# Expert stage: the relu rows change partition quarters through memory, and the second product runs two tiles behind the first

## The reference

```
logits = x @ w_gate;  expert = argmax(logits);  gate = softmax(logits)[expert]
for e in range(8):
    xe  = x[tokens of e]                      # rows gathered by expert
    h   = maximum(xe @ w1[e], 0)              # 512 -> 1024
    out[tokens of e] = gate * (h @ w2[e])     # 1024 -> 512
```

## Time and profile before

| what | value |
|---|---|
| median of 3 runs | 1513.52 us (1509.26 to 1514.18) |
| the profiled execution, its own time | 1509.39 us |
| its span, first to last instruction | 1507.7 us |
| PE busy | 98% of the span |
| DVE, ACT, POOL busy | 65%, 47%, 42% |
| expert stage, first product of tile 3 to the end | 1058.6 to 1507.7 us |

### The profile page before, as it was taken

The page is one execution under the profiler, slowest core; times in us unless marked ns, Lnnn a source line. Parts: engine busy times, 40 slices in busy tenths (PEclk is TensorE's granted clock), DMA queues, the critical chain, the costliest instruction groups (busy, mean ns, idle before and its releaser), DMA issues.

```text
span 1507.7 us, 28846 instructions
## 1 busy us (share of the span) xinstructions
PE 1473.6 (98%) x8070; PEld 1274.8 (85%) x8071; DVE 979.4 (65%) x1877; ACT 713.0 (47%) x1512; POOL 630.7 (42%) x681
## 2 busy tenths in 40 slices
PE   7999999999999999999999999999999899999997
PEld 6999999999978888888888888887888778888885
DVE  5688888888825374655637465535677777777663
ACT  5688788788812122121212212143566566656442
POOL 6676676676810021020202102021667776665221
PEclk9999999999999999999999999999999999999999
DMA  7354344344430202021120202134424433321110
GB/s 254 115 142 107 104 107 107 103 108 127 109 122 0 71 15 84 0 84 28 56 70 14 84 0 84 29 131 153 167 96 141 163 116 130 125 73 49 40 48 23
DMA packets 84601, 134.67 MB, mean 89 GB/s; under 512 B 50016, under 2 KB 50272, under 8 KB 80338
## 3 DMA queue, kind: packets, MB, share of 16 engines
q1 hardware_dynamic: 76978, 114.01, 25.2%
q0 software_dynamic: 7584, 20.17, 4.2%
HBM read 104.26 MB, written 30.94 MB: 90 GB/s over the span
## 4 chain that ended last, share of the span: by engine, by line
PE 67%; DVE 1%; DMA 1%; POOL 1%; issue 1%; ACT 1%; POOLq 0%; ACTq 0%; DVEq 0%
PE bank L166 65%; PE bank L1669 1%; POOL big L1104 1%; DVE xs L1466 1%; DMA arena<-rows_scratch,ids 1%; ACT arena L1244 0%; DMA out<-arena,ids 0%; DVE arena L1451 0%; PE bank L1600 0%; PE bank L1705 0%; PE bank L1619 0%; PE bank L1608 0%; ACT big L809 0%; PE bank L1594 0%; DVE xs L1428 0%
## 5 line engine op out<-in xcount | busy, mean ns | idle before, releaser
L166 PE MATMUL bank<-big,xs 128*128 (+1 forms) x2088 | 492.6, 395 | 14.7 <-DVE big L609 8.1
L166 PEld LDWEIGHTS bank<-big,xs 128*128 128x128 f32 x2088 | 391.7, 189 | 96.7 <-issue 15.8
L166 PE MATMUL bank<-xs,big 128*128 128x512 f32 x1728 | 397.4, 391 | 2.7 <-PEq L215 2.7
L166 PEld LDWEIGHTS bank<-xs,big 128*128 128x128 f32 x1728 | 324.7, 188 | 70.3 <-issue 2.9
L166 PE MATMUL bank<-big 128*128 128x512 f32 (+1 forms) x1632 | 325.8, 348 | 2.0 <-POOL big L305 1.4
L166 PEld LDWEIGHTS bank<-big 128*128 128x128 f32 (+1 forms) x1632 | 255.8, 165 | 36.2 <-POOL big L305 1.7
L1021 POOL TENSOR_TENSOR arena<-arena 128x512 f32<-128x512 f32 x32 | 39.8, 1255 | 440.5 <-DMA arena<-rec_scratch 440.2
L1397 DVE TENSOR_TENSOR arena<-arena,bank 128x512 f32<-128x512 f32 x72 | 49.4, 686 | 246.0 <-PE bank L166 246.0
L1157 ACT COPY arena<-bank 128x512 f32<-128x512 f32 x72 | 42.3, 587 | 306.9 <-PE bank L166 302.6
L1322 DVE CUSTOM_DVE_ANT_0 arena<-arena 128x512 f32<-128x512 f32 x256 | 159.5, 688 | 14.9 <-ACT arena L1177 14.7
L1451 DVE TENSOR_SCALAR arena<-bank,gate 32x256 f32<-32x256 f32 x288 | 138.9, 482 | 44.5 <-PE bank L166 40.1
(11 more groups left out here) (175 smaller groups left out, 1395.0 us busy)
## 6 DMA issues: line engine op xcount, KB each, us to landing
arena<-we SPq DMA_DIRECT2D x32, 1024.0 KB, 4.8
kqraw<-kq SPq DMA_DIRECT2D x32, 576.0 KB, 3.8
rows_scratch<-arena SPq DMA_DIRECT2D x36, 256.5 KB
xT_scratch<-arena SPq DMA_DIRECT2D x32, 288.0 KB
arena<-v SPq DMA_DIRECT2D x64, 128.0 KB, 2.4
arena<-xT_scratch SPq DMA_DIRECT2D x8, 1024.0 KB, 5.4
arena<-rec_scratch SPq DMA_DIRECT2D x64, 128.0 KB, 3.8
arena<-w3T SPq DMA_DIRECT2D x8, 512.0 KB, 3.4
```

Of the source, the lines that this page charges most:

```text
L166: ins = nc.tensor.matmul(out, left[a], right[b], start=first and n == 0, stop=last and n == 2)
```

## The change

The relu is again one instruction per half on ACT, with partitions in place. `relu_stored(g)` then stores the 128 x 1024 rows to a scratch tensor in HBM (512 KB, one DMA issued by ACT), and `load_quarters(g)`, later in ACT's tile, waits for the store and issues four loads of 128 KB, each of 32 partitions x (4 x 256 columns), which bring the quarters to their places in `hq`. DVE turns the rows of tile g - 1 in tile g, and PE's second product in tile g is that of g - 2. The weight subtraction of the loop moves from POOL to DVE, at the end of DVE's tile; POOL's tile is a gather and a scatter. ACT's chunks move to the end of its tile, behind the loads. The table of chunks is worked out anew for the longer distance. In the prologue second product(1) and the transposes of tile 2 go; in the tail PE makes first product(39), second product(37) with the transposes of tile 39 between its halves, `last_product` (tile 39, its parts in buffers of its own), and then second product(38).

```diff
+            def relu_stored(g):
+                for h in range(2):
+                    relu_half(g, h, True)
+                act.wait_ge(relu_done[0], g + 1)
+                act.dma_start(m["hrows"][ds(g * P, P), :], hs).then_inc(h_stored, 16)
+
+            def load_quarters(g):
+                act.wait_ge(h_stored, 16 * g + 16)
+                stored = m["hrows"][ds(g * P, P), :].rearrange("(b i) (a c) -> a i b c", i=Q, a=P // Q)
+                for a in range(P // Q):
+                    act.dma_start(hq[a * Q:(a + 1) * Q, :].rearrange("i (b c) -> i b c", b=P // Q), stored[a]
+                                  ).then_inc(hq_in, 16)
...
             def tile(g):                       # ACT
-                relu_moved(g)
+                relu_stored(g)
                 rows_high(g + 1, False)
+                next_gate(g + 1)
+                turned_h_high(g - 1)
+                load_quarters(g)
                 tile_chunks(act, g, weights)
-                next_gate(g + 1)
-                turned_h_high(g)
...
             def tile(g):                       # DVE
-                relu_moved(g)
-                turn_h(g)
-                result(g - 1)
-                turned_h_low(g)
+                rows_low(g + 1)
+                turn_h(g - 1)
+                result(g - 2)
+                turned_h_low(g - 1)
+                tile_chunks(dve, g, weights)
...
             def period(g):                     # POOL
                 gather(g + 2)
-                tile_chunks(pool, g, weights)
-                scatter(g - 1)
+                scatter(g - 2)
...
             def tile(g):                       # PE
-                here, before = weights_of(g), weights_of(g - 1)
+                here, before = weights_of(g), weights_of(g - 2)
                 for h in range(2):
                     first_product(g, h, *here)
                 x_transpose(g + 1)
-                second_product(g - 1, *before)
+                second_product(g - 2, *before)
...
+            pe.wait_ge(ht_lo, 2)               # PE, prologue
             h_transpose(1)
 
             for h in range(2):
                 first_product(2, h, 0, 0)
             x_transpose(3)
-            second_product(1, 0, 0)
-            h_transpose(2)
+            second_product(0, 0, 0)
...
-            second_product(g1, *before, between=lambda: h_transpose(g))
-            second_product(g, *here, out=ylast_ps, left=htlast)
+            second_product(g2, *before2, between=lambda: h_transpose(g))
+            last_product(*here)
+            second_product(g1, *before)
```

More of the change, by code:

```diff
@@ L110, in alloc @@
     over("filler", [XW], xs_at)
[L111 removed]
+    over("htlast", [2, FF // 2], arena_at + (SLOTS * CW + FF) * 4, F32R)
     def cut(*parts):
@@ L1111, in _ @@
             pool.wait_ge(tabs, 2)
[L1112 to L1115, removed]
             def period(g):
                 gather(g + 2)
-                tile_chunks(pool, g, weights)
-                scatter(g - 1)
+                scatter(g - 2)
             last = tiles(pool, period, 2)
-            last1, last2 = last_of(pool, 1), last_of(pool, 2)
             keep_gate(last)
[L1125 to L1130, removed]
+            scatter(last_of(pool, 3))
+            scatter(last_of(pool, 2))
+            row = table(m, pool, ROW, last, 0, E * TPE)
+            pool.tensor_copy(m["idg"][:], m["idall"][:, ds(row, 1)]).then_inc(idg_set, 1)
+            pool.wait_ge(idg_set, last + 2)
+            pool.wait_ge(last_sb, 1)
+            pool.sem_inc(turn_taken, 1)
+            pool.indirect_dma_start(t["out"], bass.IndirectOffsetOnAxis(m["idg"][:, 0:1], 0), ylast, None,
+                                    bounds_check=N - 1, oob_is_err=False).then_inc(last_out, 16)
+            scatter(last_of(pool, 1))
+            pool.wait_ge(last_out, 16)
+            pool.wait_ge(scattered, 16 * last)
         @block.scalar
@@ L1559, in _ @@
+            linked(dve.scalar_tensor_tensor(ahead_of[:, most], ex[:, back], early_w2, ex[:, one], ALU.add, ALU.max), base)
+            linked(dve.scalar_tensor_tensor(ch[:, most], ahead_of[:, most], early_w2, ch[:, most], ALU.add, ALU.max), base)
             linked(dve.tensor_scalar(ch, ch, float(CPE), float(NCH), ALU.mult, ALU.min), base)
@@ L1683, in first_product, with second_product @@
                 last.then_inc(h_mm, 1)
-            def second_product(g, e, base, between=None, out=y_ps, left=ht):
-                if out is y_ps:
-                    pe.wait_ge(y_sb, g + 1)
+            def second_product(g, e, base, between=None):
+                pe.wait_ge(y_sb, g + 1)
                 for j in range(FC):
@@ L1694, in second_product, with last_product @@
                         pe.wait_ge(ht_lo, 2 * g + j // DC + 1)
-                    last = split3(nc, out[:], parts(left[:, :, j]),
+                    last = split3(nc, y_ps[:], parts(ht[:, :, j]),
                                   parts(ring[:, :, ds(base + (W1C * CW + j * DM), DM)]), j == 0, j == FC - 1)
                 last.then_inc(y_mm, 1)
+            def last_product(e, base):
+                pe.wait_ge(w_lo, CPE * e + CPE)
+                for j in range(FC):
+                    pe.wait_ge(last_lo, j // DC + 1)
+                    last = split3(nc, ylast_ps[:], parts(htlast[j // DC][:, :, j % DC]),
+                                  parts(ring[:, :, ds(base + (W1C * CW + j * DM), DM)]), j == 0, j == FC - 1)
+                last.then_inc(last_mm, 1)
             def h_transpose(g):
```

160 lines of the change are left out of this document (81 added, 79 removed).

## The result

| what | before | after |
|---|---|---|
| median of 12 runs each, us | 1511.36 (1506.70 to 1514.18) | 1520.38 (1515.61 to 1527.87) |
| ratio to before, with its 95% interval | | 1.0063 (1.0045 to 1.0081) |
| span of the profiled execution, us | 1507.7 | 1513.9 |

The forecast was 4.3 us less than before. The medians differ by 9.0 us the other way. The range of 1503 to 1532 holds the time, but it does so for reasons that the forecast didn't have.

A forecast was written before the change was run, and what follows sets the result against it. PE, busy 98% of the span, was taken as the bound. The span summed as 1507.7 - 11.2 (loop) + 2.2 (prologue and tail) + 4.7 (two-chunk waits) = 1503.4 us, giving a median of 1509.2; range 1503 to 1532.

The forecast's parts named there:

- A: Whole kernel: the forecast itself, 1509.2 us, own range 1503 to 1514 for clock drop and two-chunk waits; chance 0.50.
- C: ACT between cast of h and weight cast: DMA issues become the new bound, 1522 or 1543 us; chance 0.24.
- D: Loop: the store lands later than 4.75 us after issue, each us over costing 23; 1526 at 5.5; chance 0.10.
- POOL's relief, 11.2 us: Loop: with the weight subtraction off POOL, its meeting with DVE and the late scatter go; up to 11.2 us back.
- Prologue, -3.2: Before the loop: first product(3) starts 3.2 us earlier despite a PE idle of 3.2; no clock drop in the sum.
- Tail, +5.5: After the loop: second product(38) adds 5.46 us; what stands after PE's last product stays.
- ACT's order in tiles with one chunk: Loop: issues run beneath the cast of turned h, then weight cast, relu, store, rows cast; slack 0.5 us.
- Two-chunk tiles, 3 x 1.6: Tiles 13, 15, 16: rows_low stands behind DVE's second subtraction, PE waits 1.6 us each, 4.7 in all.
- B: Loop: two-chunk waits vanish too, because ACT is earlier than summed; 1504.5 us; chance 0.08.
- The store's landing: Loop: ACT's loads wait for it; taken as 3.4 us after issue, with 4.25 allowed, 4.75 with the slack.
- E: Single-tile expert: stalls only move, weights or a gather still come late; 1513 to 1520 us; chance 0.08.
- What would show it: Timeline signs: tiles of 11.36 us but for 13, 15, 16; rows_low waits mark C or D; none for turned h.

The follow-up runs named there:

- the prologue's edit: Changed kernel with second product(0) put ahead of the transposes of tile 3 in the prologue; 1519.05 us, 1.0071 of the kernel before.
- the tail's edit: Changed kernel with PE reading the tail's tile and expert numbers before the loop; 1523.17 us, 1.0087 of the kernel before.
- the first of the better versions: Changed kernel: casts before loads, second product(0) before tile 3's transposes, POOL's first subtraction awaiting the tables, shorter tail reads; 1506.35 us, 0.9968 of before.

## Why the prediction was wrong

The step that failed most is ACT's order in and behind the tiles with two chunks. The prediction let the store land 3.4 us after its issue in every tile, so that the four loads never wait for it, and it put what the two-chunk tiles lose down to DVE's order. In three tiles the loads began 6.7 to 8.0 us after the store, and in all of them what was due stood behind the loads. The loop lost 12.9 us and not 4.7, and 9.7 of them came back when the casts went ahead of the loads. Beside that the prologue was off by 2.8 us and the tail by 2.0. The forecast's own range (A) ended at 1514. That the wider one held the time is luck: rivals that weren't there (C) or in three tiles only (D) had widened it. Term by term:

- **POOL's relief, 11.2 us:** right. The weight subtraction back on POOL costs 11.4 us of the loop.
- **Prologue, -3.2:** the idle was sized right (3.22) and the step "I take none and keep 2.7 for the range" failed: the clock fell and took 2.5 us. With the slower transposes (0.77 us to the next product instead of 0.35) that is all of the 2.8 us by which the term was off. The bracket had an idle of 1.96 without and one of 3.86 with a fall, and 3.2 is nearer the upper end; "full work before it" was no reason that any row showed.
- **Tail, +5.5:** 2.0 us too small. 1.4 are the reads of the table for three tiles, which the change adds ahead of first product(39) and which I didn't count; moved, they are gone. The other 0.6 lies behind PE's last product, from its end to the end of the span (11.9 us, before 11.2), where the prediction had that "what stands after PE's last product stays". Of it 0.5 is behind the issue of the last scatter, which now carries tile 38 (0.26 MB) and not the partly empty tile 39 (0.06). That the bytes are the cause is argued, not shown.
- **ACT's order in tiles with one chunk:** mechanism right, slack mis-sized: 0.5 forecast, -0.07 measured. The four issues end 0.4 us later than summed, the reads after them take 1.75 instead of 1.6. It cost little, some 0.7 us over all such tiles.
- **Two-chunk tiles, 3 x 1.6:** 2.1, 2.3 and 1.7 us with the landings out of the way, 6.1 instead of 4.7. The reason given against B, that DVE's subtractions stand in order whatever ACT does, is wrong: without the loads ahead of the casts the waits vanish (0.2 us left).
- **The store's landing:** "I take 3.4: the next weight load is asked for only when DVE's subtraction has ended, after the store's issue" holds for the tiles with one chunk or none, where no load waited for its store (in tile 15, with no weight load about, it had landed within 3.3 us). In a two-chunk tile the first of DVE's two subtractions ends ahead of the store's issue, at T + 7.35 + 2.3 = T + 9.65 by the prediction's own times, with the store at T + 8.85 + 1.91 = T + 10.8; so in tiles 14, 16 and 17 a weight load stands 0.2 to 0.3 us before it, the landing takes 6.7 to 8.0 us, and that cost about 3.7 us. The upper end of 4.8 came from a load by itself, not from a store behind one. The prediction's fit from the Trainium skill, "DMA: Bandwidth & Descriptors", section "Anatomy of one DMA", is given there for transfers issued by GpSimd, which the prediction doesn't say; its estimate of 3.2 us agrees with tile 15 and says nothing of the three.
- **Gathers:** two came late to PE (0.65 and 1.24 us), and behind the second, and the 2.43 that followed, came 1.6 us of low clock. Which of the two idles brought it isn't shown: in the runs with a quarter of the bytes and with the prologue's edit it came behind 2.24 and 2.47 alone. The late gathers are E's mechanism in a small size; it wasn't in the sum. With the three points above it makes up the loop's 8.3 us, though not as a clean sum, since a wait removed also removes the fall of the clock behind it.
- **The rivals:** C had the side right, not the mechanism: the issues cost 0.33 to 0.39 us and ran beneath the cast. D had the mechanism, in three tiles and not in 20. E was there, too. The clock in the prologue was kept for A's range and left out of the sum, the reads in the tail are nowhere: together 3.9 of the 13.2 us between forecast and result.

What would show it was put right: PE's waits on `rows_low` in the tiles named, late loads behind a store as D's mark, and no wait for the turned h.

## What to carry to other kernels

A transfer whose latency is hidden can still cost, if its issue waits in an engine's order ahead of work that is due: put the wait for a landing behind the work that doesn't need it (one line moved gave back 9.7 us here). Take the landing time from the tile in which a large load is asked for just ahead of the transfer, not from the median, and work out for every kind of tile which of the two is asked for first. Before a product that stands between two waits is moved, see what it covers on both sides, and count table reads in PE's queue as work when nothing is queued ahead of them.

## What the runs showed of the hardware

The length of an idle alone didn't tell whether PE's clock would fall. In the expert stage of these runs it fell after every idle of 3.16 us and more, and between 1.96 and 2.52 both happened. It fell after 1.97, 1.98 (the tail's edit), 2.10 (POOL's subtraction), 2.24, 2.37, 2.39, 2.43 and 2.47 us. It didn't after 1.96 (before), 1.98 (a quarter of the bytes, the prologue's edit), 2.01, 2.02, 2.15 (POOL's subtraction), 2.28 (before, ahead of the transposes of tile 2) and 2.52 (the first of the better versions). Two idles of the run with small weight loads:

```profile
1193.52 5.73 PE L167 MATMUL bank<-big,xs 128*128 x24 [2.02 <-DVE xs L1452]
1218.49 7.35 PE L167 MATMUL bank<-big,xs 128*128 x24 [1.97 <-DVE xs L1452]
```

The fall cost 1.6 us there (7.35 instead of 5.73 for 24 products), 2.5 in the changed kernel's prologue and 2.7 in the loop before.

POOL's issue of a gather took 2.5 to 3.1 us instead of 0.99 in 13 of the loop's tiles, each time begun 0.08 to 0.65 us after a subtraction of a chunk on DVE. Where the subtraction began with the issue or behind it, the issue stayed at 0.99. Before, with the subtraction on POOL, no issue was slow. POOL's timeline, then DVE's, of the changed kernel:

```profile
1178.02 3.08 POOL L1063 DMA_INDIRECT arena<-rows_scratch,idg  x1 [0.84 <-POOL idg L1060]
```

```profile
1177.94 2.29 DVE L1486 TENSOR_TENSOR big<-arena,big  x1 [4.07 <-ACT big L810]
```

This gather landed 9.6 us after its issue (3.4 in the median before) and is the one that PE waited for at 1187.69. The other one that PE waited for, and both in the run with the casts ahead of the loads, had slow issues too (2.72 us); most slow ones kept nobody waiting. So the subtraction's move from POOL to DVE took POOL's time away and left a little of the meeting. And the table step of 0.19 us that took 5.0 to 5.4 beside POOL's subtraction is the same meeting the other way round. The Trainium skill, "SBUF — State Buffer", section "SBUF: two separate sides", has one of the two engines blocked for the whole instruction of the other when both need the pair of ports that they share, and whichever starts first gets it. The trace agrees for that step, which in the run with the prologue's edit ends at 1048.52, POOL's at 1048.46. By the profile the step begins 0.69 us ahead of the subtraction, while POOL still issues a gather, so what it stood behind at first isn't shown.
